# Decay-gated attention with a routed and a dense feed-forward: the first loads in another order, a norm moved to VectorE, and two transposes moved to idle PSUM banks

## The reference

```python
# attention with a decayed state: B, H, S, D = 4, 8, 768, 48
for t in range(S):
    state = alpha[:, :, t, :, None] * state + np.einsum('bhd,bhe->bhde', k[:, :, t], v[:, :, t])
    y[:, :, t] = np.einsum('bhd,bhde->bhe', q[:, :, t], state)
x = np.ascontiguousarray(attn_out.transpose(0, 2, 1, 3)).reshape(B * S, H * D)
# experts: N, D, E, F = 3072, 384, 8, 1024; each row goes to one of eight
en = expert_emb / (np.linalg.norm(expert_emb, axis=-1, keepdims=True) + 1e-06)
logits = xn @ en.T / tau
...
    h = np.maximum(x[mask] @ w1[e], 0.0)
    out[mask] = gate_w[mask, None] * (h @ w2[e])
# dense feed-forward, d_ff = 768
h = np.maximum(np.maximum(x @ w1, x @ w2), x @ w3)
return (h @ w_out).astype(np.float32)
```

## Time and profile before

| | us |
|---|---|
| median of 3 runs | 816.65 |
| lowest, highest | 816.34, 819.27 |
| the profiled execution's own time | 816.65 |
| span of its instructions | 814.9 |
| TensorE busy in the span | 757.6 |
| VectorE, ScalarE, GpSimd busy | 373.7, 284.0, 244.0 |

### The profile page before, as it was taken

How to read it: one execution, slowest core, us unless ns; L and a number is a source line. 1 busy time by engine, 2 the same in 40 slices (tenths; PEclk the granted TensorE clock), 3 DMA queues, 4 the chain that set the end, 5 groups by cost and what they waited for, 6 DMA issues and landing times.

```text
span 814.9 us, 15765 instructions
## 1 busy us (share of the span) xinstructions
PE 757.6 (93%) x4804; PEld 663.3 (81%) x4805; DVE 373.7 (46%) x703; ACT 284.0 (35%) x635; POOL 244.0 (30%) x154
## 2 busy tenths in 40 slices
PE   2988998989389999999999998999999999999998
PEld 2877887878269999999999886888888888888887
DVE  6767786866763343424244224333333323333322
ACT  5757777774422232222223222321222212222110
POOL 3143342420137457537284495100000000000000
PEclk9989999999699999999999999999999999999999
DMA  9999887960659054432333103001101011000001
GB/s 142 240 137 162 109 109 129 116 117 2 247 183 339 26 198 144 168 133 107 125 109 123 40 22 90 27 20 40 39 19 40 20 39 39 10 19 10 10 20 48
DMA packets 128882, 75.76 MB, mean 93 GB/s; under 512 B 102648, under 2 KB 122112, under 8 KB 128832
## 3 DMA queue, kind: packets, MB, share of 16 engines
q1 hardware_dynamic: 119632, 54.88, 30.9%
q0 software_dynamic: 3328, 10.23, 4.0%
q10 hardware_dynamic: 5872, 10.03, 3.4%
HBM read 59.00 MB, written 16.12 MB: 92 GB/s over the span
## 4 chain that ended last, share of the span: by engine, by line
PE 85%; SPq 4%; issue 3%; DVE 3%; DMA 2%; ACT 2%; POOL 0%; ACTq 0%; DVEq 0%
PE bank L1353 64%; PE bank L1152 4%; SPq L300 4%; PE bank L1245 3%; PE bank L1389 3%; PE bank L1234 2%; PE bank L1182 2%; PE bank L1213 2%; DMA nat<-in_alpha 1%; PE bank L1226 1%; PE bank L1339 1%; PE bank L1200 1%; PE bank L1425 1%; DVE Sm L837 1%; ACT sq L591 1%
## 5 line engine op out<-in xcount | busy, mean ns | idle before, releaser
L461 POOL TENSOR_TENSOR wsp<-raw,wsp 128x1536 f32 x28 | 103.8, 3725 | 92.9 <-DVE wsp L1044 92.9
L1353 PE MATMUL bank<-yh,mh 128*128 128x512 f32 x324 | 128.2, 396 | 0.6 <-issue 0.6
L1353 PE MATMUL bank<-yh,ml 128*128 128x512 f32 x324 | 126.4, 390 | 0.0
L1353 PE MATMUL bank<-yl,mh 128*128 128x512 f32 x324 | 91.2, 390 | 0.0
L1353 PE MATMUL bank<-wsp,xh 128*128 (+1 forms) x324 | 85.2, 398 | 3.7 <-issue 3.7
L1353 PE MATMUL bank<-wsp,hTh 128*128 x432 | 81.5, 339 | 1.3 <-ACT hTh L694 1.3
L502 POOL DMA_INDIRECT yg<-expert_rows,pos_i x24 | 24.5, 1020 | 172.0 <-ACT ygs L731 164.9
L750 ACT CAST gh<-t 128x512 fp32r<-128x512 f32 x36 | 22.3, 621 | 152.7 <-DVE t L1117 152.7
L1353 PEld LDWEIGHTS bank<-wsp,hTh 128*128 128x128 f32 x432 | 73.6, 188 | 1.5 <-issue 1.5
L1353 PEld LDWEIGHTS bank<-wsp,xh 128*128 128x128 f32 x324 | 58.9, 188 | 16.1 <-issue 4.9
L1353 PEld LDWEIGHTS bank<-yl,mh 128*128 128x128 f32 x324 | 60.8, 188 | 13.0
(11 more groups left out here) (197 smaller groups left out, 1320.8 us busy)
## 6 DMA issues: line engine op xcount, KB each, us to landing
raw<-in_moe_w SPq DMA_DIRECT2D x16, 1536.0 KB, 8.0
expert_rows<-ye ACTq DMA_DIRECT2D x27, 192.0 KB, 3.6
nat<-in_alpha SPq DMA_DIRECT2D x32, 144.0 KB, 3.2
nat<-in_k SPq DMA_DIRECT2D x32, 144.0 KB, 3.9
nat<-in_q SPq DMA_DIRECT2D x32, 144.0 KB, 4.3
vt<-in_v SPq DMA_DIRECT2D x32, 144.0 KB, 4.5
attention_rows<-xc SPq DMA_DIRECT2D x4, 1152.0 KB, 6.3
out<-oo SPq DMA_DIRECT2D x24, 192.0 KB
```

The costliest lines, as they stand in the source:

```text
L461: g.tensor_tensor(wsp[:, ds(to, 1), 1, n, part], raw[:, n:n + 1, part], wsp[:, ds(to, 1), 0, n, part].bitcast(f32), ALU.subtract).then_inc ...
L1353: last = mm(o, x, y, start=(n == 0), stop=(n == len(todo) - 1))
```

## The change

SP no longer loads the embeddings and tau: ScalarE issues these two before its table load. SP starts at once with the attention loads, and for units 0 to 3 it issues them by tensor in the order (unit, tensor) that the loop lists: alpha 0, alpha 1, k 0, q 0, alpha 2, k 1, q 1, v 0 and so on. The loads of units 4 to 15 keep their order. The one semaphore `kqv_in` of a buffer becomes `k_in`, `q_in` and `v_in`, so TensorE waits for each by itself.

The squares, their sum and the root of the embeddings' norm are now made on VectorE. `near_root` halves the exponent by a shift and an added constant and makes two Heron steps, and `exact_norm` makes the last one as before. The padding of buffers 2 and 3 goes from VectorE to GpSimd (`late_pads`).

In the prologue, alpha of unit 1 is turned into banks 4 and 5 and that of unit 2 into banks 6 and 7; before, both used banks 0 and 1. ScalarE copies alpha of unit 1 directly behind that of unit 0. VectorE copies the identity into `read` ahead of its first scans, and does `scans(1, 1)` ahead of `recip(0, 0)`.

```diff
@@ -288,17 +288,18 @@
-        sp.dma_start(embn[:], emb).then_inc(emb_in, 16)
-        sp.dma_start(tau_sb[:], tau.rearrange("(a b) -> a b", a=1).to_broadcast([P, 1])).then_inc(tau_in, 16)
+        def load_one(u, j, n, slow=None):
+            for h in range(2):
+                to = nat[j][:, n, :, h, 0:D] if n < 3 else vt[j][:, :, h, 0:D]
+                s = (alpha, k, q, v)[n].rearrange("b h (c p) d -> (b h) p c d", p=P)[ds(2 * u + h, 1)]
+                sp.dma_start(to, s.rearrange("o p c d -> p (o c) d")).then_inc(
+                    slow or (alpha_in, k_in, q_in, v_in)[n][j], 16)
...
-            for n, src in enumerate((alpha, k, q, v)):
-                for h in range(2):
-                    to = nat[j][:, n, :, h, 0:D] if n < 3 else vt[j][:, :, h, 0:D]
-                    s = src.rearrange("b h (c p) d -> (b h) p c d", p=P)[ds(2 * u + h, 1)]
-                    sp.dma_start(to, s.rearrange("o p c d -> p (o c) d")).then_inc(
-                        slow or (kqv_in if n else alpha_in)[j], 16)
+            for n in range(4):
+                load_one(u, j, n, slow)
@@ -307,8 +308,10 @@
-        for j in range(UPB):
-            load(j, j)
+        for j, n in ((0, 0), (1, 0), (0, 1), (0, 2), (2, 0), (1, 1), (1, 2), (0, 3),
+                     (3, 0), (2, 1), (1, 3), (2, 2), (2, 3), (3, 1), (3, 2), (3, 3)):
+            load_one(j, j, n)
@@ -399,6 +402,10 @@
+        for j in range(2, NAT):
+            g.memset(nat[j][:, 0, :, :, D:HL], 1.0)
+            g.memset(nat[j][:, 1:3, :, :, D:HL], 0.0)
+            g.memset(vt[j][:, :, :, D:HL], 0.0).then_inc(late_pads, 1)
@@ -509,18 +516,16 @@
-        act.wait_ge(emb_in, 16)
-        a.activation(sq[0:E, :], embn[:], ACT.Square, accum_out=es[:, 0:1]).then_inc(achain, 1)
-        act.wait_ge(achain, 1)
-        a.activation(es[:, 1:2], es[:, 0:1], ACT.Sqrt).then_inc(e_act, 1)
+        act.dma_start(embn[:], emb).then_inc(emb_in, 16)
+        act.dma_start(tau_sb[:], tau.rearrange("(a b) -> a b", a=1).to_broadcast([P, 1])).then_inc(tau_in, 16)
...
-        def stage_a(u, j):
+        def stage_a(u, j, b0=0):
...
-                a.copy(halves(aT[j % 2], h), cols(bank[h], h)).then_inc(act_a, 1)
+                a.copy(halves(aT[j % 2], h), cols(bank[b0 + h], h)).then_inc(act_a, 1)
@@ -607,11 +612,11 @@
+        stage_a(1, 1, 4)
...
-        stage_a(1, 1)
+        stage_a(2, 2, 6)
+        stage_a2(1, 1)
...
-        stage_a2(1, 1)
-        stage_a(2, 2)
@@ -785,12 +790,25 @@
-        for j in range(NAT):
+        for j in range(2):
...
-        dve.wait_ge(e_act, 1)
+        def near_root(out_, square, y, r):
+            link(d.tensor_scalar(y.bitcast(i32), square.bitcast(i32), 1, None, ALU.logical_shift_right))
+            link(d.tensor_scalar(y.bitcast(i32), y.bitcast(i32), 0x1FBD1DF5, None, ALU.add))
+            for n in range(2):
+                link(d.reciprocal(r, y))
+                link(d.tensor_tensor(r, r, square, ALU.mult))
+                link(d.tensor_tensor(y, y, r, ALU.add))
+                link(d.tensor_scalar(out_ if n else y, y, 0.5, None, ALU.mult))
+        dve.wait_ge(emb_in, 16)
+        link(d.tensor_tensor(sq[0:E, :], embn[:], embn[:], ALU.mult))
+        link(d.tensor_reduce(es[:, 0:1], sq[0:E, :], AX.X, ALU.add))
+        near_root(es[:, 1:2], es[:, 0:1], es[:, 2:3], es[:, 3:4])
@@ -865,17 +883,17 @@
+        dve.wait_ge(ident_ready, 1)
+        for jj in range(UPB):
+            d.tensor_copy(read[:, jj, 0:P], ident[:])
...
-            d.tensor_copy(read[:, jj, 0:P], ident[:])
...
+        scans(1, 1)
...
-        scans(1, 1)
@@ -1143,7 +1161,7 @@
-        pe.wait_ge(pads_ready, NAT)
+        pe.wait_ge(pads_ready, 2)
@@ -1152,12 +1170,12 @@
-        def turn_alpha(u, j):
+        def turn_alpha(u, j, b0=None):
...
-                if not (isinstance(u, int) and u < 2):
+                if b0 is None:
...
-                turn(u, j, 0, h, bank[h], pe_a)
+                turn(u, j, 0, h, bank[(b0 or 0) + h], pe_a)
@@ -1189,6 +1207,7 @@
+                pe.wait_ge(q_in[j1], 32 * (b + (1 if j >= 3 else 0)) + 32)
@@ -1205,6 +1224,7 @@
+            pe.wait_ge(v_in[j], 32 * b + 32)
@@ -1246,29 +1266,33 @@
-                pe.wait_ge(kqv_in[j2], 96 * (b + (1 if j >= 2 else 0)) + 96)
+                pe.wait_ge(k_in[j2], 32 * (b + (1 if j >= 2 else 0)) + 32)
...
-        turn_alpha(0, 0)
+        turn_alpha(0, 0, 0)
...
+        pe.wait_ge(alpha_in[1], 32)
+        turn_alpha(1, 1, 4)
+        pe.wait_ge(k_in[0], 32)
+        turn_k(0, 0)
+        pe.wait_ge(q_in[0], 32)
...
-        pe.wait_ge(alpha_in[1], 32)
-        turn_alpha(1, 1)
-        pe.wait_ge(kqv_in[0], 96)
-        turn_k(0, 0)
...
+        pe.wait_ge(late_pads, NAT - 2)
...
-        turn_alpha(2, 2)
+        pe.wait_ge(e_copy, 1)
+        turn_alpha(2, 2, 6)
...
-        pe.wait_ge(kqv_in[1], 96)
+        pe.wait_ge(k_in[1], 32)
...
-        pe.wait_ge(e_copy, 1)
+        pe.wait_ge(dve_qp, CR + 2)
```

More of the change, by code:

```diff
@@ L212, in new @@
         return [sem[n] for n in names]
-    ident_ready, pads_ready = new("ident_ready", "pads_ready")
+    ident_ready, pads_ready, late_pads = new("ident_ready", "pads_ready", "late_pads")
     const_ready, tau_in, emb_in, gconst = new("const_ready", "tau_in", "emb_in", "gconst")
     alpha_in = new(*[f"alpha_in{j}" for j in range(NAT)])
-    kqv_in = new(*[f"kqv_in{j}" for j in range(NAT)])
+    k_in, q_in, v_in = (new(*[f"{n}_in{j}" for j in range(NAT)]) for n in "kqv")
     pe_a, pe_k, pe_q, pe_kT, pe_S, pe_U, pe_Y = new("pe_a", "pe_k", "pe_q", "pe_kT", "pe_S", "pe_U", "pe_Y")
@@ L223, in build @@
     act_yT, pe_X, act_X, act_ss, x_out = new("act_yT", "pe_X", "act_X", "act_ss", "x_out")
-    dchain, achain = new("dve_chain", "act_chain")
-    e_act, e_dve, e_pe, e_copy = new("emb_act", "emb_dve", "emb_pe", "emb_copy")
+    (dchain,) = new("dve_chain")
+    e_dve, e_pe, e_copy = new("emb_dve", "emb_pe", "emb_copy")
     r_ss, r_sqrt, r_hot, r_cnt, r_sh, r_ex, r_1h, r_inv, r_tab, r_gate, r_high, r_tile = new(
```

## The result

| | before | changed |
|---|---|---|
| median of 20 runs each, us | 817.25 | 820.88 |
| lowest, highest | 816.17, 820.28 | 818.84, 825.86 |
| the profiled execution's own time, its span | 816.65, 814.9 | 823.84, 822.0 |
| mean granted clock of TensorE in it | 0.979 | 0.969 |
| start of the alpha of unit 4 on TensorE | 45.06 | 43.66 |

The ratio is 1.0045, with an interval of 1.003 to 1.0059: slower by 3.7 us, where 815.8 was forecast. The profiled execution of the changed kernel lies at the slow end of its runs, so its 7.2 us over the one before are taken apart first and weighed against the medians afterwards.

The account below looks back on a forecast made before the run. It took SP's issue queue, then the transfer of unit 4's alpha, then TensorE as the bound. Only the small loads' -0.88 counted, other terms 0: 816.65 - 0.88 = 815.8 us, range 815.2 to 816.3.

Parts of the forecast that it names:

- The split waits: TensorE's separate waits for q_in and v_in in each of 16 units: taken as 0, ends 0 and +5.4 us.
- The third rival: TensorE pays 5.4 us for the added waits in its units, giving 821.2 us; chance 0.03.
- signs of being wrong: Alpha of unit 4 before 42 or after 45, TensorE reaching it after 42, or a mid-batch unit above 10.7 us.
- The clock: Behind 60 us, batch boundaries included: every piece expected the same, some 0.9 us earlier.
- The second rival: Third batch boundary turns cold, its pieces at the slow clock: 817.4 us, slower than before; chance 0.15.
- The small loads: SP's queue at the start: attention loads and alpha of unit 4 come earlier, -0.88 us, bounds 0 and -1.68.
- The order: New load order for units 0 to 3: data come at other times, stream end unchanged; worth 0.
- The norm: Embeddings' norm on VectorE at the start: ends at 9.2 against 7.43, scans begin up to 1.8 us later.
- The banks: Prologue: first mask at 21.8, 3.8 us earlier, lost in a 6.2 us wait for unit 4's alpha; worth 0.
- The clock at the alpha: Slow stretch on TensorE from 45.06 to 51.35, at unit 4's alpha: taken as 0, bounds 0 and -1.2 us.

Follow-up runs that it names:

- run 5: Changed kernel with eight more bare semaphore increments at the head of TensorE's list: 816.22 us, ratio 0.9997.
- run 10: Changed kernel with eight fewer bare semaphore increments on TensorE and ScalarE's squares at inner batch boundaries over 48 columns, not 384: 808.74 us, ratio 0.988.
- run 1: Changed kernel with eight of TensorE's bare semaphore increments taken out of the last two units: 818.55 us, ratio 1.0006.
- Run 3: Kernel before with only the two small loads (embeddings, tau) moved from SP to ScalarE: 817.1 us, ratio 0.9992.
- run 4: Changed kernel with eight fewer bare semaphore increments and the loads of units 0 to 3 unit by unit again: 818.72 us, ratio 1.0008.
- run 8: Changed kernel with eight fewer bare semaphore increments and the first expert's weights in 11 pieces behind the loads of units 4 to 7: 809.29 us, ratio 0.9898.
- run 7: Kernel before with the first expert's weights in 11 pieces behind the loads of units 4 to 7, GpSimd's splits one batch later: 811.6 us, ratio 0.9928.
- 11: Changed kernel, all its increments kept, with ScalarE's squares at inner batch boundaries over 48 columns, not 384: 812.49 us, ratio 0.9934.
- run 2: Kernel before with eight more bare semaphore increments at the head of TensorE's list: 822.17 us, ratio 1.0061.
- run 6: Kernel before with three more small loads into an unused buffer at the head of SP's queue: 820.56 us, ratio 1.0026.

## Why the prediction was wrong, point by point

*The step that failed* is "The split waits ... I take 0, with 0 and +5.4 as ends". Their own time was indeed nothing: from unit 0's last product to unit 1's is 10.62 us now (26.58 to 37.20) and was 10.63. But the step counted a wait as a wait only. Each is also an instruction in the code, eight in all ahead of the router, and these moved a pause of 3.9 us out of the shadow of a 10-us wait onto the path. The third rival priced waits at 821.2, which is 0.3 us from the result, with 0.03 of chance. That is luck, and so is it that 3.9 lies within the step's own ends of 0 and +5.4: both price a wait at the issue of each, and run 5 refutes that, with eight instructions more, all waits kept, and 816.22.

None of the prediction's signs of being wrong came: the alpha of unit 4 stands at 43.66 (between 42 and 45), TensorE reaches it at 38.7, and a unit takes 10.62 us. All of them look at the first 60 us, and the loss lies behind.

*The clock* was the second miss. "Behind 60 us every piece is the same, some 0.9 us earlier" does not hold: it fails at the first boundary. The second rival was right in kind, the third boundary did turn slow in the profiled execution (the earlier trace rows against 175.95), and too small: three boundaries changed, and cost 4.5 us there. In the medians it is less. The whole difference is +3.6; with 3.9 for the pause and -1.2 for the start (-1.09 to -1.40 at the alpha, -1.18 in run 10) some 0.9 us are left. That these are slow stretches that come more often is argued and not shown: the same remainder is 2.8 us in run 1 (1.5 above the kernel before, with the alpha 1.36 earlier) and 0.4 in run 5 (1.2 below, with the alpha 1.64 earlier).

*The small loads*, -0.88: the alpha of unit 4 came 1.40 us earlier, inside the step's bounds of 0 and -1.68. Between 30 and 33 us the engines now move 240 GB/s for 120, and a new hole stands at 28 us (25 GB/s). Run 3 alone gives -1.09. The mechanism was right and the size low by 0.2 to 0.5.

*The order, worth 0*: right (run 4). *The norm*, done at 9.58 for 9.2: right, and hidden. *The banks*: the mask at 22.52 for 21.8, a head start of 3.12 us for 3.8, a wait of 4.96 for 6.2; worth 0, right, and for the reason given, as run 8 against run 7 shows. What the step did not see is the second chain that ends beside the first: GpSimd starts on the weights at 42.53 in both kernels, although they are issued 1.03 us earlier in the changed one. In run 3, with the old order, it starts at 41.16.

*The clock at the alpha*, 0: right for the profiled executions; the six transposes take 1.54 us in both kernels.

## What to carry to other kernels

A change that adds or drops instructions anywhere in an engine's list moves all code behind it, and can bring a pause like this one, most likely in the delivery of instructions, onto the path. When a trace shows several microseconds of "issue" between two neighbouring instructions that wait for nothing, shift the code by a few bare instructions and measure again before blaming the change. A head start in front of a wait for a transfer is worth nothing until that transfer moves, so move the bulk load behind it first. And when runs fall into groups, compare at equal mean granted clock: it told a gain of 1 us that the medians hid. Mind that idle time counts in that mean, so a pause shifts it.

## What the runs showed that was not expected

- A shift of 8 instructions costs 3.75 us (11 against 10) to 5.1 us (2 against before), and a shift of 16 costs nothing.
- The same three products in sequence at a batch boundary run at 0.50 or at 1.00 of the clock after a wait of about 2 us, from one execution to the next. Low mean clocks were more frequent both with a start 1 us later (run 6) and with one 1.4 us earlier (run 1), while run 5, as early as run 1, had them about as rarely as the kernel before. In run 2, with no earlier start, the third boundary of the profiled execution was slow as well. What decides it is open, and with 12 runs each the shares are rough.
